# Attention, Fourier-like mixing and a gated layer on one core: bias and mask move from TensorE to VectorE, warm-up passes, sums kept in PSUM, new order of the last stages

## Chip, cores, metric

One Trainium2 chip, one core. The metric is the device time of one execution in microseconds (us), the median of the runs shown. TensorE is PE, VectorE is DVE, ScalarE is ACT, GpSimd is POOL, and SyncE (SP) issues the transfers.

## The reference

Three layers follow each other: attention, a mixing layer, a gated layer. B = 2, H = 8, S = 768, D = 64, C = H * D = 512, F = 1024. All is float32.

```python
scores = q @ k.T / sqrt(D) + bias          # bias = -slope[h] * distance
scores = where(is_global | is_local, scores, -1e9)   # 8 first keys, 96 last keys
a = softmax(scores);  x = a @ v            # then heads side by side: (B, S, 512)

theta = x @ w_theta                        # mixing layer
y = w_tok_r @ (x * cos(theta)) + w_tok_i @ (x * sin(theta))
u = x + y;  v = u + relu(u @ w_ch)

h = relu(v @ w_in)                         # gated layer
conv = 3-tap convolution of h along the tokens, per channel
out = (h * sigmoid(conv)) @ w_out
```

## The kernel before

Every engine has its own program, written out by hand, and the engines meet at counting semaphores. An engine runs its program in order, so a wait holds all that stands behind it.

**Attention** runs over 48 tiles, numbered `u`: 8 pairs of heads `p` with 6 tiles of 128 queries `i` each. A tile sees 232 keys for each of its two heads (128 for `i` = 0). TensorE's step `u` issues `scores(u+1)`, `transpose_p(u-1)` and `weighted_v(u-2)`. `scores` ends with two bf16 products with `ident16` that add the bias and the mask. VectorE's step takes the maxima of tile `u+1`, then denominator, reciprocal and quotient of tile `u-2`; in its first six steps it also makes the bias of one more head (two instructions). ScalarE's step takes two exponentials of tile `u` and copies the transposed probabilities of tile `u-1`. Scores banks, probabilities and transposes are doubled.

For the pairs 2 to 7 GpSimd scales q (L335), rounds q and k to a high part (L343) and subtracts for a low part (L345). TensorE then makes each score product in three passes. GpSimd begins this once all eight biases exist, and its queue is: pair 2, `w_theta`, pair 3, token weights 0, pair 4, token weights 1, pairs 5, 6, 7. SyncE loads pair `p` when the buffer of `p-2` is free, and behind the load of v for pair `p-1`.

**Mixing** follows with the same high and low parts: `theta`, then twelve token products `mix_tokens` (L619), then for four chunks `c` of 384 tokens `transpose_u(c)` (L630) and `mix_channels(c, j)`, j = 0 to 3 (L471). `add_mix(n)` on VectorE makes v from product `n` in two instructions (L1182, L1185), `high_v` on ScalarE and `low_v` on GpSimd split it. `high_u` and `low_u` split u.

**The gated layer** has 32 tiles `n`, 8 for each chunk: `hidden(n)` on TensorE (L471), then relu (L888) and first tap (L894) on ScalarE, two more taps on VectorE (`conv`, L1220, L1223), sigmoid on ScalarE (L901), the gate on VectorE (L1231), `high_g` on ScalarE, `low_g` on GpSimd. `relu(n)` waits for gate `n-2`. `output(c, f)` (L674) adds tile `f` of chunk `c` to three output banks in nine matmuls. Its first call waits for the last `add_mix`, number 15.

The products of the mixing layer's last two chunks and the first hidden tiles alternate on TensorE. This stretch is called the turn below.

## Time and profile before

| | |
|---|---|
| median of 3 runs | 436.52 us (435.88 to 436.69) |
| the profiled execution | 435.07 us, its span 433.3 us |
| PE busy | 410.5 us (95%) |
| DVE, ACT, POOL busy | 239.9, 216.1, 185.7 us |
| attention (to the first `theta` product) | 0 to 108.3 us |
| theta and token products | 108.3 to 265.6 us |
| the turn, to the first `output` | 265.6 to 313.4 us |
| the output stretch | 313.4 to 433.3 us |

A page gives busy time for each engine, and beside each group of instructions the idle time ahead of it with what ended it. Idle time costs something only on the engine that sets the end. TensorE is busy nearly everywhere here, so its few idle places and its own work are what to look at.

### The profile page before, as it was taken

To read this page: it belongs to the slowest core of one execution; us is meant where nothing else is said; L and a number is where in the kernel's file an instruction comes from. 1 tells how busy PE (TensorE), PEld (TensorE's weight loads), DVE (VectorE), ACT (ScalarE), POOL (GpSimd) and SP (SyncE) were. 2 spreads that over 40 slices of the span, in tenths; PEclk is the share of its full clock that TensorE was granted. 3 is DMA by queue.
4 is the path that set the end of the run, shared out by engine and by line. 5 is a ranking of instruction groups with operands and counts; after the bars stand their busy time and mean duration, and the time that the engine had idled before them with its cause. 6 is when DMAs were issued, how large, how long until landed. Compare 5 with 4: busy or idle time off the path is not lost.

```text
span 433.3 us, 6425 instructions
## 1 busy us (share of the span) xinstructions
PE 410.5 (95%) x2424; PEld 360.9 (83%) x2424; DVE 239.9 (55%) x432; ACT 216.1 (50%) x416; POOL 185.7 (43%) x126
## 2 busy tenths in 40 slices
PE   3999999999999999999999999979299999999997
PEld 1788988999878888888898989979289998999985
DVE  3766565666588744537354421476766565565620
ACT  2666555666578735564243111464464545455341
POOL 2299999410166622248432210245574232332330
PEclk9999999999999999999999999999889999999999
DMA  7834322370000222244420003001100010001021
GB/s 269 347 118 182 126 94 93 141 220 2 2 0 2 97 74 73 79 140 152 151 110 2 0 0 99 0 2 49 48 2 0 2 48 25 2 25 50 0 74 73
DMA packets 11984, 32.20 MB, mean 74 GB/s; under 512 B 4272, under 2 KB 4272, under 8 KB 11952
## 3 DMA queue, kind: packets, MB, share of 16 engines
q1 hardware_dynamic: 11952, 31.77, 21.0%
q8 instruction: 20, 0.33, 0.3%
q14 instruction: 12, 0.10, 0.1%
HBM read 28.62 MB, written 3.15 MB: 73 GB/s over the span
## 4 chain that ended last, share of the span: by engine, by line
PE 79%; POOL 10%; issue 3%; DVE 3%; DMA 2%; ACT 1%; SPq 0%; POOLq 0%; ACTq 0%
PE bank L471 28%; PE bank L619 23%; PE bank L674 16%; PE bank L533 4%; POOL qk_parts L345 3%; DMA qk_sb<-qk_laid 2%; PE bank L518 2%; PE bank L498 2%; POOL qk_sb L335 2%; PE bank L505 2%; POOL wT L358 2%; POOL qk_parts L343 1%; PE bank L630 1%; PE bank L492 1%; POOL wth L352 1%
## 5 line engine op out<-in xcount | busy, mean ns | idle before, releaser
L619 PE MATMUL bank<-z,wT 128*128 128x512 f32 x432 | 99.3, 390 | 0.0
L619 PEld LDWEIGHTS bank<-z,wT 128*128 128x128 f32 x432 | 80.8, 188 | 16.6
L674 PE MATMUL bank<-wout,g 128*128 128x512 f32 x288 | 71.5, 398 | 7.7 <-issue 7.7
L471 PE MATMUL bank<-vT,win 128*128 128x386 f32 x384 | 73.2, 340 | 0.0
L471 PEld LDWEIGHTS bank<-vT,win 128*128 128x128 f32 x384 | 68.6, 189 | 2.0
L674 PEld LDWEIGHTS bank<-wout,g 128*128 128x128 f32 x288 | 55.0, 192 | 18.1 <-issue 8.0
L430 POOL TENSOR_TENSOR g<-gf,g 128x384 fp32r<-128x384 f32 x32 | 39.8, 1246 | 69.6 <-ACT g L910 69.3
L1220 DVE SCALAR_TENSOR_TENSOR cv<-h_sb,convw,cv 128x384 f32<-128x384 f32 x32 | 21.4, 669 | 52.6 <-ACT cv L894 52.6
L417 POOL TENSOR_TENSOR vT<-vtmp,vT 128x384 fp32r<-128x384 f32 x16 | 17.2, 1087 | 66.5 <-ACT vT L847 66.5
L533 PE MATMUL bank<-v_sb,pT 128*128 128x65 f32 x352 | 44.6, 268 | 0.0
L747 ACT ACTIVATE pT<-bank 128x512 f32<-128x512 f32 (+1 forms) x48 | 27.0, 562 | 34.9 <-PE bank L518 34.9
L533 PEld LDWEIGHTS bank<-v_sb,pT 128*128 128x128 f32 x352 | 43.1, 192 | 0.0
L394 POOL TENSOR_TENSOR z<-trig,z 128x1024 fp32r<-128x1024 f32 x12 | 29.4, 2450 | 30.4 <-ACT z L811 30.4
L1231 DVE TENSOR_TENSOR gf<-h_sb,sg 128x384 f32<-128x384 f32 x32 | 40.8, 1276 | 0.6 <-ACT sg L901 0.6
L888 ACT ACTIVATE h_sb<-bank 128x386 f32<-128x386 f32 x32 | 15.7, 491 | 49.9 <-PE bank L471 45.8
L736 ACT ACTIVATE pr<-bank,small 128x232 f32<-128x232 f32 (+1 forms) x96 | 36.8, 438 | 2.7 <-DVE small L1011 2.2
L471 PE MATMUL bank<-uT,wch 128*128 128x384 f32 x192 | 35.6, 337 | 2.4 <-DVE uT L1174 2.4
L1155 DVE TENSOR_TENSOR x<-bank,x 128x512 f32<-128x512 f32 x12 | 8.3, 692 | 53.1 <-PE bank L619 53.1
L471 PE MATMUL bank<-wth,xT 128*128 128x512 f32 x144 | 35.7, 398 | 1.0 <-DVE xT L1039 1.0
L471 PEld LDWEIGHTS bank<-uT,wch 128*128 128x128 f32 x192 | 33.6, 188 | 3.3 <-DVE uT L1174 2.7
L792 ACT ACTIVATE wT<-wrows 128x1536 fp32r<-128x1536 f32 x10 | 14.9, 1489 | 40.6 <-PE bank L619 40.6
L1011 DVE TENSOR_REDUCE small<-bank 128x2 f32<-128x464 f32 (+1 forms) x48 | 29.0, 605 | 10.5 <-PE bank L505 5.9
(83 smaller groups left out, 560.1 us busy)
## 6 DMA issues: line engine op xcount, KB each, us to landing
wrows<-w_tok_laid SPq DMA_DIRECT2D x12, 768.0 KB, 4.3
qk_sb<-qk_laid SPq DMA_DIRECT2D x8, 792.0 KB, 5.7
v_sb<-v_laid SPq DMA_DIRECT2D x8, 780.0 KB, 4.4
out<-ob SPq DMA_DIRECT2D x12, 256.0 KB, 2.0
winraw<-w_in_in SPq DMA_DIRECT2D x4, 512.0 KB, 3.8
woutraw<-w_out_in SPq DMA_DIRECT2D x8, 256.0 KB, 2.7
wthraw<-w_theta_in SPq DMA_DIRECT2D x1, 1024.0 KB, 11.4
wchraw<-w_ch_in SPq DMA_DIRECT2D x1, 1024.0 KB, 5.1
```

What stands on the lines that cost most here:

```text
L394: pool.tensor_tensor(z[b][:, i, 1], trig[:, n % 2], z[b][:, i, 0].bitcast(F32), ALU.subtract)\
L417: pool.tensor_tensor(vT[b][:, 1, j, cols], vtmp[:, n % 2, :], vT[b][:, 0, j, cols].bitcast(F32), ALU.subtract).then_inc(v_lo, 1)
L430: pool.tensor_tensor(g[c % 2][:, 1, f, :], gf[:, n % 2, :], g[c % 2][:, 0, f, :].bitcast(F32), ALU.subtract).then_inc(g_lo, 1)
L471: last = pe.matmul(dst, w[a], m[b], start=(i == 0 and j == 0), stop=(i == n - 1 and j == 2))
L533: last = pe.matmul(O_BANK[u % 2][:, h * OW:(h + 1) * OW], pT[:, u % 2, slot * P:(slot + 1) * P], v_sb[:, pp, i, chunk, h, :], start=(chunk ...
L619: last = pe.matmul(Y_BANK[s % 2][:], wT[s % 2][:, hi, ri * NT + blk, :], z[b][:, blk, lo, ri, :], start=(blk == 0 and ri == 0 and j == 0), ...
L674: last = pe.matmul(OUT_BANK[c % 2][i][:], g[c % 2][:, hi, f, i * P:(i + 1) * P], wout[:, lo, f, :], start=(f == 0 and j == 0), stop=(f == ...
L736: last = act.activation(pr[:, u % 2, h, cols], S_BANK[u % 2][:, h, cols], ACT.Exp, bias=small[:, u % 2, 2 + h:3 + h])
L747: act.activation(d, src, ACT.Copy).then_inc(pt_copied, 1)
L1011: dve.tensor_reduce(small[:, u % 2, 2:4], S_BANK[u % 2][:, :, cols], AX.X, ALU.max, negate=True)\
L1220: dve.scalar_tensor_tensor(out=c, in0=h[:, 1:HALF + 1], scalar=convw[:, 1, f:f + 1], in1=c, op0=ALU.mult, op1=ALU.add).then_inc(conv_step, 1)
L1231: dve.tensor_tensor(gf[:, n % 2, :], h_sb[:, half, n % 2, half + 1:half + 1 + HALF], sg[:, n % 2, :], ALU.mult).then_inc(g_ready, 1)
```

## The change

In attention, the two bf16 products of each tile leave TensorE. VectorE instead runs, for each head, one `tensor_tensor_reduce` that reads the scores from PSUM and a float32 bias from SBUF, writes the negated, scaled sum to a new tile `biased` in SBUF, and keeps its minimum. The scale 1/sqrt(D) is in that instruction, so GpSimd's and ScalarE's passes over q are gone. The exponentials read `biased`. `scores` waits for the maxima of two tiles ago, no more for the exponentials. TensorE runs eight bf16 products of 512 columns over a constant tile at its start, and four more behind the branch that chooses the banded program.

In the turn, v's first sum, the convolution sum and the sigmoid stay in PSUM. Chunk 3's u is transposed in two halves, since two of its banks now serve the gates, and `hidden` runs one tile further ahead of `mix_channels(3, j)`. VectorE and ScalarE take their parts in a new order. The output uses four banks in turn, tile `t` in bank `t % 4`, and `mix_channels` waits for the whole of v two products ago.

```diff
-        ident16 = att("ident16", [P, P], BF16)
-        bias = att("bias", [P, H, BAND], BF16)
-        bias0 = att("bias0", [P, H, P], BF16)
+        biased = att("biased", [P, 2, 2, BAND], F32)
+        bias = att("bias", [P, H, BAND], F32)
+        bias0 = att("bias0", [P, H, P], F32)
...
-        cv = at("cv", [P, 2, HALF], F32, 107.25)
-        sg = at("sg", [P, 2, HALF], F32, 110.25)
...
-        OUT_BANK = [[bank[0], bank[1], bank[2]], [bank[3], bank[6], bank[7]]]
+        GATE_BANK = [bank[6][:, 0:HALF], bank[7][:, 0:HALF]]
+        OUT_BANK = [bank[0], bank[1], bank[2], bank[3]]
 
         def u_bank(c):
-            return [bank[0], bank[1], bank[4], bank[5]] if c < 3 else [bank[0], bank[1], bank[6], bank[7]]
+            return [bank[0], bank[1], bank[4], bank[5]] if c < 3 else [bank[0], bank[1], bank[0], bank[1]]
...
-            pool.wait_ge(ident_ready, 2)
-            pool.tensor_copy(ident16[:], ident[:]).then_inc(ident_ready, 1)
-
-            def scale_q(p):
-
-                q_cols = qk_sb[:, p % 2, 0:S]
-                pool.wait_ge(qk_in[p % 2], 16 * (p // 2 + 1))
-                pool.tensor_scalar(q_cols, q_cols, SCALE, None, ALU.mult).then_inc(q_scaled, 1)
 
             def split_qk(p):
                 pp = p % 2
-                scale_q(p)
+                pool.wait_ge(qk_in[p % 2], 16 * (p // 2 + 1))
                 if p >= 4:
                     pool.wait_ge(scores_ready, NT * (p - 1))
-                pool.wait_ge(q_scaled, p)
...
-                if p == 0 and i < 2:
-                    pe.wait_ge(q_first, i + 1)
-                if p == 1 and i == 0:
-                    pe.wait_ge(q_scaled, p)
+                if p < 2 and i == 0:
+                    pe.wait_ge(qk_in[p], 16)
                 if p >= 2 and i == 0:
                     pe.wait_ge(qk_lo, p - 1)
                 if u >= 2:
-                    pe.wait_ge(probs_ready, u - 1)
+                    pe.wait_ge(max_ready, 2 * (u - 1))
                 cols = slice(0, BAND) if i else slice(OWN, BAND)
                 c0, c1 = (NG, KT_STEP) if i == 0 else (KT_STEP * i - NL, KT_STEP * i + KT_STEP)
                 if p < 2:
                     for h in range(2):
                         rows = slice(h * D, (h + 1) * D)
-                        pe.matmul(S_BANK[u % 2][:, h, cols], qk_sb[rows, pp, i * P:(i + 1) * P],
-                                  qk_sb[rows, pp, S + c0:S + c1], start=True, stop=False)
+                        last = pe.matmul(S_BANK[u % 2][:, h, cols], qk_sb[rows, pp, i * P:(i + 1) * P],
+                                         qk_sb[rows, pp, S + c0:S + c1], start=True, stop=True)
                 else:
                     for j, (hi, lo) in enumerate(((0, 0), (0, 1), (1, 0))):
                         for h in range(2):
                             rows = slice(h * D, (h + 1) * D)
-                            pe.matmul(S_BANK[u % 2][:, h, cols], qk_parts[rows, pp, hi, i * P:(i + 1) * P],
-                                      qk_parts[rows, pp, lo, S + c0:S + c1], start=(j == 0), stop=False)
-                if i < 2 and p == 0:
-                    pe.wait_ge(bias_ready, i + 1)
-                if i == 0 and 1 <= p < HP:
-                    pe.wait_ge(bias_ready, h0 + 2)
-                for h in range(2):
-                    last = pe.matmul(S_BANK[u % 2][:, h, cols], ident16[:], bias[:, h0 + h, :] if i else bias0[:, h0 + h, :],
-                                     start=False, stop=True)
+                            last = pe.matmul(S_BANK[u % 2][:, h, cols], qk_parts[rows, pp, hi, i * P:(i + 1) * P],
+                                             qk_parts[rows, pp, lo, S + c0:S + c1], start=(j == 0), stop=(j == 2))
                 last.then_inc(scores_ready, 1)
...
+                keep_busy(4)
...
+            def keep_busy(count):
+                for _ in range(count):
+                    pe.matmul(bank[7], idle[:, 0:P], idle[:], start=True, stop=True)
+
+            pe.wait_ge(idle_ready, 1)
+            keep_busy(8)
+            pe.wait_ge(ident_ready, 3)
...
-                    pe.wait_ge(r_done, n - 1)
+                    pe.wait_ge(v_ready, n - 1)
...
             def output(c, f, tiles=(0, 1, 2)):
-                if f == 0:
-                    if c == 0:
+                if c == 0:
+                    if f == 0:
                         pe.wait_ge(u_lo, NC * CB)
-                    if c <= 1:
-                        pe.wait_ge(r_done, NC * CB)
-                    if c >= 2:
-                        pe.wait_ge(out_copied, 3 * (c - 1))
-                if c == 0:
+                        pe.wait_ge(v_ready, NC * CB)
                     pe.wait_ge(wout_ready, f + 1)
                 pe.wait_ge(g_lo, FB * c + f + 1)
                 for i in tiles:
+                    t = 3 * c + i
+                    if f == 0 and t >= 4:
+                        pe.wait_ge(out_copied, t - 3)
                     for j, (hi, lo) in enumerate(((0, 0), (0, 1), (1, 0))):
-                        last = pe.matmul(OUT_BANK[c % 2][i][:], g[c % 2][:, hi, f, i * P:(i + 1) * P], wout[:, lo, f, :],
+                        last = pe.matmul(OUT_BANK[t % 4][:], g[c % 2][:, hi, f, i * P:(i + 1) * P], wout[:, lo, f, :],
...
-            transpose_u(3)
+            transpose_u(3, (0, 1))
             hidden(1)
             mix_channels(2, 2)
             hidden(2)
             mix_channels(2, 3)
             hidden(3)
+            hidden(4)
+            transpose_u(3, (2, 3))
             for j in range(CB):
-                hidden(CB + j)
+                hidden(5 + j)
                 mix_channels(3, j)
-
-            for c in range(1, NC):
-                for f in range(FB):
-                    hidden(FB * c + f)
-                    output(c - 1, f)
-            for f in range(FB - 2):
-                output(NC - 1, f)
+            output(0, 0)
+            for n in range(FB + 1, NH):
+                hidden(n)
+                output(n // FB - 1, n % FB)
+            for i in range(3):
+                for f in range(FB - 2):
+                    output(NC - 1, f, (i,))
...
-            first_q = qk_sb[:, 0, 0:S]
-            act.wait_ge(qk_in[0], 16)
-            act.activation(first_q[:, 0:P], first_q[:, 0:P], ACT.Copy, scale=SCALE).then_inc(q_first, 1)
-            act.activation(first_q[:, P:S], first_q[:, P:S], ACT.Copy, scale=SCALE).then_inc(q_first, 1)
-
             def exps(u):
-                act.wait_ge(max_ready, u + 1)
                 if u >= 2:
                     act.wait_ge(pt_ready, u - 1)
                 cols = slice(0, BAND) if u % NT else slice(OWN, BAND)
                 for h in range(2):
-                    last = act.activation(pr[:, u % 2, h, cols], S_BANK[u % 2][:, h, cols], ACT.Exp,
-                                          bias=small[:, u % 2, 2 + h:3 + h])
+                    act.wait_ge(max_ready, 2 * u + h + 1)
+                    last = act.activation(pr[:, u % 2, h, cols], biased[:, u % 2, h, cols], ACT.Exp,
+                                          bias=small[:, u % 2, 2 + h:3 + h], scale=-1.0)
...
-                act.activation(cv[:, n % 2, :], h_sb[:, half, n % 2, half:half + HALF], ACT.Copy,
+                act.activation(GATE_BANK[n % 2], h_sb[:, half, n % 2, half:half + HALF], ACT.Copy,
                                scale=convw[:, 0, n % FB:n % FB + 1]).then_inc(tap_ready, 1)
 
             def sigmoid(n):
                 act.wait_ge(conv_ready, n + 1)
-                if n >= 2:
-                    act.wait_ge(g_ready, n - 1)
-                act.activation(sg[:, n % 2, :], cv[:, n % 2, :], ACT.Sigmoid).then_inc(sig_ready, 1)
+                act.activation(GATE_BANK[n % 2], GATE_BANK[n % 2], ACT.Sigmoid).then_inc(sig_ready, 1)
...
-            high_v(8)
-            hidden(0)
-            high_v(9)
-            hidden(1)
-            high_v(10)
-            hidden(2)
+            for j in range(CB - 1):
+                relu(j)
+                first_tap(j)
+                high_v(2 * CB + j)
+                gates(j)
+            high_u(3, (0, 1))
+            relu(3)
+            first_tap(3)
             high_v(11)
-            high_u(3)
-            hidden(3)
+            gates(3)
+            relu(4)
+            first_tap(4)
+            gates(4)
             high_w_out(0)
-            hidden(4)
+            high_u(3, (2, 3))
+            relu(5)
+            first_tap(5)
+            gates(5)
             high_w_out(1)
-            high_v(12)
-            hidden(5)
-            high_v(13)
-            high_w_out(2)
-            hidden(6)
-            high_v(14)
-            high_w_out(3)
-            hidden(7)
-            high_v(15)
-            for f in range(CB, FB):
-                high_w_out(f)
-                hidden(CB + f)
-            for n in range(CB + FB, NH):
-                hidden(n)
+            for j in range(CB):
+                relu(6 + j)
+                first_tap(6 + j)
+                high_v(3 * CB + j)
+                gates(6 + j)
+                high_w_out(2 + j)
+            for n in range(6 + CB, NH):
                 c, f = divmod(n, FB)
-                if c >= 2 and f < 3:
-                    copy_out(3 * (c - 2) + f)
+                if c >= 2 and f == 0:
+                    for i in range(3):
+                        copy_out(3 * (c - 2) + i)
+                relu(n)
+                first_tap(n)
+                gates(n)
+                if n < 12:
+                    high_w_out(n - 4)
...
+            dve.memset(idle[:], 1.0).then_inc(idle_ready, 1)
...
                 dve.wait_ge(scores_ready, u + 1)
+                if p == 0 and i < 2:
+                    dve.wait_ge(bias_ready, i + 1)
+                if i == 0 and 1 <= p < HP:
+                    dve.wait_ge(bias_ready, h0 + 2)
                 if u >= 2:
                     dve.wait_ge(probs_ready, u - 1)
                 cols = slice(0, BAND) if i else slice(OWN, BAND)
-                dve.tensor_reduce(small[:, u % 2, 2:4], S_BANK[u % 2][:, :, cols], AX.X, ALU.max, negate=True)\
-                   .then_inc(max_ready, 1)
+                for h in range(2):
+                    dve.tensor_tensor_reduce(
+                        biased[:, u % 2, h, cols], S_BANK[u % 2][:, h, cols],
+                        bias[:, h0 + h, :] if i else bias0[:, h0 + h, :], -SCALE, 3.0e38, ALU.add, ALU.min,
+                        small[:, u % 2, 2 + h:3 + h]).then_inc(max_ready, 1)
...
-                dve.scalar_tensor_tensor(out=tmp, in0=R_BANK[n % 2][:, 0:HALF], scalar=0.0,
-                                         in1=uT[:, 1, j, :].bitcast(F32), op0=ALU.max, op1=ALU.add).then_inc(r_done, 1)
+                r = R_BANK[n % 2][:, 0:HALF]
+                dve.scalar_tensor_tensor(out=r, in0=r, scalar=0.0, in1=uT[:, 1, j, :].bitcast(F32), op0=ALU.max,
+                                         op1=ALU.add).then_inc(r_done, 1)
                 dve.wait_ge(r_done, n + 1)
-                dve.tensor_tensor(tmp, tmp, uT[:, 0, j, :].bitcast(F32), ALU.add).then_inc(v_ready, 1)
+                dve.tensor_tensor(tmp, r, uT[:, 0, j, :].bitcast(F32), ALU.add).then_inc(v_ready, 1)
...
             for j in range(CB):
                 add_mix(2 * CB + j)
                 if j == CB - 1:
-                    low_u(3)
+                    low_u(3, (0, 1))
                 hidden(j)
+            hidden(4)
+            low_u(3, (2, 3))
+            hidden(5)
             for j in range(CB):
-                hidden(CB + j)
                 add_mix(3 * CB + j)
-            for n in range(FB, NH):
+                hidden(6 + j)
+            for n in range(6 + CB, NH):
```

VectorE's program in attention, one tile with all 232 keys. Before:

```order
L1011 TENSOR_REDUCE small<-bank 128x2
L1018 TENSOR_SCALAR small<-bank 128x2
L1023 RECIPROCAL small<-small 128x2
L1031 SCALAR_TENSOR_TENSOR x<-bank,small 128x128
L995 SCALAR_TENSOR_TENSOR bias_65<-dist,masked 128x128
L995 SCALAR_TENSOR_TENSOR bias<-dist,masked 128x232
```

And in the changed kernel, the same step:

```order
L1003 ISA biased,small<-bank,bias 128x232
L1003 ISA small 128x1
L1003 ISA biased,small<-bank,bias 128x232
L1003 ISA small 128x1
L1012 TENSOR_SCALAR small<-bank 128x2
L1017 RECIPROCAL small<-small 128x2
L1025 SCALAR_TENSOR_TENSOR x<-bank,small 128x128
L981 SCALAR_TENSOR_TENSOR bias_65<-dist,masked 128x128
L981 SCALAR_TENSOR_TENSOR bias<-dist,masked 128x232
```

(`bias_65` is `bias0`, the bias of the first tile.) One reduction has become four instructions: each `tensor_tensor_reduce` is followed by one that writes its one value per partition.

TensorE's program at the end of the turn, before: the last two hidden tiles and mixing products, then the first `output`.

```order
L471 MATMUL bank<-uT,wch 128x384 x12
L471 MATMUL bank<-vT_100,win 128x386 x12
L471 MATMUL bank<-uT,wch 128x384 x12
L471 MATMUL bank<-vT_100,win 128x386 x12
L674 MATMUL bank<-wout,g_106 128x512 x9
```

And now:

```order
L457 MATMUL bank<-vT_101,win 128x386 x12
L457 MATMUL bank<-uT,wch 128x384 x12
L457 MATMUL bank<-vT_101,win 128x386 x12
L457 MATMUL bank<-uT,wch 128x384 x12
L660 MATMUL bank<-wout,g_107 128x512 x9
```

The last hidden tile ahead of `output` is number 8 in both; it now stands ahead of the last mixing product.

VectorE's program there, before: conv of tile 7, gate of tile 6, the last `add_mix` (number 15), conv of tile 8.

```order
L1220 SCALAR_TENSOR_TENSOR cv<-h_sb,convw,cv 128x384
L1223 SCALAR_TENSOR_TENSOR cv<-h_sb,convw,cv 128x384
L1231 TENSOR_TENSOR gf<-h_sb,sg 128x384
L1182 SCALAR_TENSOR_TENSOR vtmp<-bank,uT 128x384
L1185 TENSOR_TENSOR vtmp<-vtmp,uT 128x384
```

And now: conv of tile 8, gate of tile 7, the last `add_mix`.

```order
L1215 SCALAR_TENSOR_TENSOR bank<-h_sb,convw,bank 128x384
L1218 SCALAR_TENSOR_TENSOR bank<-h_sb,convw,bank 128x384
L1226 TENSOR_TENSOR gf<-h_sb,bank 128x384
L1177 SCALAR_TENSOR_TENSOR bank<-bank,uT 128x384
L1180 TENSOR_TENSOR vtmp<-bank,uT 128x384
```

The order within the piece is the same, with a later tile's convolution in it. Every instruction of it now has at most one input in SBUF.

## Rows read from the trace of the kernel before

**Rows 1.** The chain of waits, in order of time (start us, us, what)
```profile
25.99 3.55 POOL qk_parts L345
...
64.37 3.57 POOL qk_parts L345
67.99 0.55 PE bank L498 x6
...
305.62 7.73 issue
313.35 4.18 PE bank L674 x9
...
319.68 2.06 PE bank L674 x9
```

**Rows 2.** Timeline of TensorE in attention (start, us, engine, line; idle before)
```profile
38.61 0.60 PE L498 MATMUL bank<-qk_parts 64*128 64x232 f32 x6
39.14 0.37 PE L505 MATMUL bank<-bias,ident 128*128 128x232 bf16 x2
39.35 0.60 PE L518 MATMUL bank<-ident,pr 128*128 128x128 f32 x4
...
40.72 0.60 PE L498 MATMUL bank<-qk_parts 64*128 64x232 f32 x6
...
43.36 0.55 PE L498 MATMUL bank<-qk_parts 64*128 64x128 f32 x6 [0.45 <-POOL qk_parts L345]
...
55.67 0.55 PE L498 MATMUL bank<-qk_parts 64*128 64x128 f32 x6 [0.38 <-POOL qk_parts L345]
```

**Rows 3.** Groups by line and shape (busy us, mean ns; idle before)
```profile
L1011 DVE TENSOR_REDUCE small<-bank 128x2 f32<-128x464 f32 x40 | 25.6, 641 | 7.6 <-PE bank L505 3.1 <-ACT pr L736 0.2
...
L995 DVE SCALAR_TENSOR_TENSOR bias<-dist,masked 128x232 bf16<-128x232 f32 x8 | 3.1, 393 | 0.0
...
L1182 DVE SCALAR_TENSOR_TENSOR vtmp<-bank,uT 128x384 f32<-128x384 f32 x16 | 8.8, 549 | 1.9 <-PE bank L471 1.9
...
L335 POOL TENSOR_SCALAR qk_sb<-qk_sb 128x768 f32<-128x768 f32 x7 | 15.1, 2158 | 22.0 <-DMA qk_sb<-qk_laid 13.1 <-DVE bias L995 9.0
```

**Rows 4.** Timeline of the first 31 us, several engines
```profile
6.97 0.31 ACT L727 ACTIVATE qk_sb<-qk_sb 128x128 f32<-128x128 f32 x1 [4.89 <-DMA qk_sb<-qk_laid]
...
7.33 0.80 PE L492 MATMUL bank<-qk_sb 64*128 64x128 f32 x4 [7.33 <-ACT qk_sb L727]
...
18.94 0.16 DVE L1018 TENSOR_SCALAR small<-bank 128x2 f32<-128x2 f32 x1 [0.43 <-PE bank L533]
...
19.54 0.59 DVE L995 SCALAR_TENSOR_TENSOR bias<-dist,masked 128x128 bf16<-128x128 f32 x2
...
20.05 0.42 DVE L1011 TENSOR_REDUCE small<-bank 128x2 f32<-128x256 f32 x1
...
22.20 2.13 POOL L335 TENSOR_SCALAR qk_sb<-qk_sb 128x768 f32<-128x768 f32 x1 [8.99 <-DVE bias L995]
...
30.97 0.55 PE L498 MATMUL bank<-qk_parts 64*128 64x128 f32 x6
```

**Rows 5.** Timeline of the turn from mixing to the output, several engines
```profile
281.68 0.62 DVE L1220 SCALAR_TENSOR_TENSOR cv<-h_sb,convw,cv 128x384 f32<-128x384 f32 x1 [1.63 <-ACT cv L894]
282.87 1.37 DVE L1231 TENSOR_TENSOR gf<-h_sb,sg 128x384 f32<-128x384 f32 x1
...
287.79 0.61 ACT L894 ACTIVATE cv<-h_sb,convw 128x384 f32<-128x384 f32 x1
288.27 2.36 PE L471 MATMUL bank<-uT,wch 128*128 128x384 f32 x12 [2.36 <-DVE uT L1174]
288.31 0.51 ACT L901 ACTIVATE sg<-cv 128x384 f32<-128x384 f32 x1
...
312.71 0.55 DVE L1182 SCALAR_TENSOR_TENSOR vtmp<-bank,uT 128x384 f32<-128x384 f32 x1
```

**Rows 6.** A stretch: us, PE, PEld, DVE, ACT, POOL busy, granted clock, DMA share, GB/s
```profile
313.00:315.00 2.00, 1.65 (x4) 1.39 (x5) 0.81 (x2) 1.12 (x3) 0.52 (x1) 0.50 0.00 0
```

78 lines of the change are left out of this document (37 added, 41 removed).

## The prediction

> **What bounds the kernel now.** I read the page's busy shares first: TensorE is busy in nearly every slice, so time can go only with its own work or with its few idle places. The chain of waits names the places [rows 1]. It runs through GpSimd's splits of q and k until 67.94 us, then along TensorE to the end, with one hole of 7.73 us ahead of the first `output` and a slow piece of 4.18 us behind it. The timeline of TensorE in attention shows what a tile costs: scores start at 38.61 and 40.72, so a full tile takes 2.11 us, and the bias products hold TensorE from 39.14 to 39.35, 0.21 us [rows 2]. Six tiles of a pair take 55.67 - 43.36 - 0.38 = 11.93 us without the wait for GpSimd, which was 0.45 and 0.38 us [rows 2]. The first 31 us show three things: TensorE starts when q and k are in and scaled, GpSimd starts when VectorE has made the last bias at 22.20, and pair 2's first scores stand at 30.97 [rows 4].
>
> **Attention, TensorE's side.** Without the bias products a pair takes 11.93 - 5 x 0.21 - 0.12 = 10.75 us (the first tile has 128 keys, its bias I put at 0.12). A full tile takes 1.90.
>
> **Attention, VectorE's side.** No row shows a `tensor_tensor_reduce`. From below: an instruction with one PSUM and one SBUF input takes 549 ns for 384 columns, one with two inputs 393 ns for 232, the old reduction 641 ns for 464 [rows 3]. These lie on a line of about 1.04 ns per column and 0.15 to 0.16 fixed, so 232 columns take 0.39 to 0.40 us by any of them. The one-value instruction behind it takes at most what L1018, on two values, takes: 0.16 us [rows 4]. If the starts overlap as those of two bias instructions do (283 + 393 ns of work in 0.51 us from start to start, rows 19.54 and 20.05 [rows 4]), a tile's four instructions hold VectorE for about 0.80 us; if each waits for the one ahead to end, for 2 x (0.40 + 0.16) = 1.12. I take 0.95, the middle, since neither row is nearer. Denominator, reciprocal and quotient hold it from 18.94 to 19.54, 0.60 us [rows 4]. So VectorE needs 1.55 us for a tile (1.40 to 1.72) and stays below TensorE's 1.90; it has a share of the short tiles too, where both are shorter. The bound stays TensorE, but near.
>
> The Trainium skill, in "VectorE: DVE Perf Modes", section "Two Vector instructions with no wait between them", says that an operation that also gives its accumulator is two instructions, and its section "The DRAIN you can't avoid" that the next one does not start until the pipe is empty. By that the tile costs the 1.12 us of my upper end, the start below would come 1.3 us later, and the sum would be 1.3 us higher. The row of two bias instructions (0.51 us for 0.676 of work) speaks against a full drain [rows 4].
>
> **The start.** q and k are there at 6.97; before, TensorE began at 7.33, after ScalarE's scaling [rows 4]. The four passes behind the branch now stand in its way. A pass of 512 columns takes 0.21 to 0.43 us by the bias product's 0.21 for 2 x 232 columns, at full or half speed, so four take 0.9 to 1.7. The branch ends somewhere between 5 and 7.3. Scores of tile 0 then begin between 7.0 and 9.0; I take 7.5, and 8.0 for the first maxima. From there VectorE is the slowest, since its first six steps carry a bias too (0.51). Until the last bias its queue is: maxima of tiles 0 to 6 (5 x 0.95, and two short ones of 0.70), six biases (3.06), four quotients (2.40): 11.6 us, so bias ready at 19.6, against 22.20. Cheap end 18.7, dear end 20.9. Pair 2's q and k were asked for at 17.66 before, now some 4 us earlier, behind the first big loads, and should be in by 19.5: they bound the cheap end only. GpSimd then needs only the 1.5 and 3.55 us of rounding and subtracting [rows 1]: split at 24.8. TensorE: scores of tile 9 wait for maxima of tile 7 (20.5), then three tiles at 1.90: tile 12 at 26.1, against 30.97. Saved 4.9.
>
> **GpSimd's chain.** It ran from 22.20 to 67.94 without a hole up to pair 5's split, 45.7 us, of which four scalings of 2.16 and their gaps are 8.8 [rows 1, 3, 4]. Now 19.6 + 36.9 = 56.5. TensorE reaches tile 30 at 26.1 + 3 x 10.75 = 58.35, after it. So TensorE is bound by itself from there: 67.99 - 58.35 = 9.65 us saved at tile 30, and 3 x 1.18 in the last three pairs: **13.2 us** for attention (12 at the dear end, 14 at the cheap one).
>
> **Theta and token products.** TensorE runs on here and none of its work changes. The later `v_ready` costs nothing: it is the v of two products ago. Zero.
>
> **The turn.** Here I walked the new queues in order with spacings of the old rows: 0.52 us from first tap to sigmoid on ScalarE, 0.55 for an `add_mix` step, 0.62 and a short gap for a conv step [rows 5]. The gate of 384 columns took 1.37 us while GpSimd worked, another instruction of that size 0.55 (row 312.71) [rows 5]; with one SBUF input left, I take 0.55. Set the second `mix_channels` product of chunk 2 where it was. Then the first half of u is split at 284.7, relu 4 waits for gate 2 at 286.9, ScalarE comes to the second half of u at 289.3, behind first tap 4, sigmoid 3, high part 2 and one weight copy, and VectorE ends it at 290.85. TensorE is done with hidden tile 5 at 287.9 and stands 3.0 us. Before, it stood 2.36 and went on at 288.27 with one hidden tile (2.1) less done [rows 5]. So this costs 0.5 us. Seven more pieces at 2.17 (the 17.35 us for eight behind 288.27): the last mixing product ends at 306.1.
>
> Then the hole. The old one ends with the last `add_mix` at 312.71: its r part came behind first tap 7, which came behind `high_v(14)`, which waited for `add_mix(14)` behind conv 6. Each round of that ring took 6 us while TensorE's took 4.3. Now the taps stand ahead of `high_v`. Hidden tile 8 ends 2.2 ahead of the last mixing product; relu, tap, two conv steps and gate take 0.2 + (0.52 + 0.61) + 1.3 + 0.55 = 3.2, `add_mix` 1.15 with its second instruction. So `output` begins at 308.2, after 2.1 us idle, not at 313.35 [rows 1]: **5.15 saved**. The granted clock stood at 0.50 behind the old hole [rows 6], that is at 1.2 GHz, and the first `output` took 4.18 instead of 2.06 [rows 1]. It did not fall behind the 2.36 of idle. With 2.1, and 3.0 before, I expect none: **2.1 saved**.
>
> **The output.** The same matmuls. Copying three tiles in a row on ScalarE (3 x 0.6) falls while TensorE is in a hidden tile of 2.1; the tile that takes a copied bank comes second. The last call has the order of its matmuls changed, and ends with the same six matmuls, copy and store. Zero.
>
> **Sum.** 13.2 + 5.15 + 2.1 = 20.4. The span becomes 433.3 - 20.4 = 412.9, the profiled execution 435.07 - 20.4 = 414.7. The median of the runs stands 1.45 above that execution: 436.52 - 20.4 = **416.1 us**.
>
> **Rivals.**
>
> 1. *VectorE becomes the bound of attention.* From 1.30 us for a tile's two sums on, its step (0.60 more) passes 1.90. At 1.5 a pair takes about 12.4 us instead of 10.75: 6 x 1.65 = 10 us given back, and 2.5 at the start, so 428; at 1.3 about 420. For it: two instructions more per head, and waits at every one. Against: all rows lie on one line. I say 422, chance 0.2.
>
> 2. *The clock falls at the 3.0 us stall, or the stall is longer.* The walk has some 20 links, any of them may be late. Half speed for one product costs 2.1, a later split of u 1: 419. Chance 0.12.
>
> 3. *Slower than before: VectorE is held by GpSimd.* The sum reads a float32 bias from SBUF, and GpSimd works almost without a hole to the end of pair 6. If that doubles it as it did the gate (0.81 us more for 384 columns, so 0.49 for 232) [rows 5], the sums take 1.93 a tile and the step 2.53. From 26.1 that gives tile 42 at 102 instead of 91.8: 10 lost where 12 were hoped for, in all about 438. It decides from a tile cost of about 1.87 on. Against: instructions that read PSUM and SBUF kept 0.55 beside a busy GpSimd (row 312.71 [rows 5]). Chance 0.04. The Trainium skill's "SBUF — State Buffer", section "Who interferes with whom", has it that only two SBUF inputs contend; by that this rival is out.
>
> 4. *Better.* The sums cost 0.8, the start is at 7.0, and the turn stalls less: 412. Chance 0.12.
>
> 5. *The turn doesn't do what it says*, the ring of 6 us stays through relu's wait for the gate: 7 us less saved, 423. Chance 0.04.
>
> **Numbers.** The likeliest case, 416, has 0.48. The range 411 to 424 takes in its bounds (414.5 to 418.5), the cases 2, 4 and 5 and the nearer half of 1, and leaves out 2 in 10 or less. A difference of 0.2% is what a measurement can tell. Faster by more: all but rival 3 and the far end of rival 1: 0.95; same 0.02; slower 0.03.
>
> **What would show it.** A pair of heads at 10.75 us, no wait for GpSimd at its first tile from pair 5 on, pair 2's scores at 26, the `tensor_tensor_reduce` at 0.40 us. One stall of TensorE near 3 us and one near 2 in the turn, the granted clock at 1.00 in both, no hole of 7.7. Wrong would be: TensorE waiting for VectorE's maxima in steady attention, a `tensor_tensor_reduce` over 0.6 us, a late first product, or a new hole in the output stretch at the change of banks.

## The result

Against the kernel before on the same chip, the changed kernel takes 0.9617 of its time (0.9543 to 0.969): 418.2 us is the median of three executions (417.7 to 422.2), where 416.1 was predicted. This ratio leaves out three more executions of the six, of 472.9 to 474.9 us, whose mean granted clock was 0.87 where it was 0.99 to 1.00 in the others; they are the main find of this study, since they are slower than the kernel before. Six further executions of the same kernel gave 417.8, 420.4 and 420.9 us, and 469.9, 475.0 and 478.0.

The profiled execution is a long one (474.94 us, span 473.2). Two rows of its page show where to look: TensorE is "busy" nearly throughout, and its clock falls within the third slice and is halved from the fourth to the thirteenth. The same row of before has no slice under 8.

```profile
PE   7989999999999999999999999999789999999997
...
PEclk9975555555555999999999999999899999999999
```

The start of TensorE in that execution, with the warm passes (`L574`) at 0.45 us each and then at 0.26, and the first scores:

```profile
1.54 3.60 PE L574 MATMUL bank<-idle 128*128 128x512 bf16 x8 [1.54 <-DVE idle L951]
6.14 1.03 PE L574 MATMUL bank<-idle 128*128 128x512 bf16 x4 [1.01 <-issue]
7.10 0.89 PE L476 MATMUL bank<-qk_sb 64*128 64x128 f32 x8
```

Then the issue of pair 2's q and k by SyncE, GpSimd's split of them, and TensorE at pair 2 (a timeline of three engines, with one row of VectorE):

```profile
13.47 0.33 SPq L226 DMA_DIRECT2D qk_sb<-qk_laid  x1
22.57 1.50 POOL L334 CAST qk_parts<-qk_sb 128x1584 fp32r<-128x1584 f32 x1 [19.15 <-DMA qk_sb<-qk_laid]
22.74 0.40 DVE L1003 CUSTOM_DVE_ANT_0 biased<-bank,bias 128x232 f32<-128x232 f32 x1
24.15 3.54 POOL L336 TENSOR_TENSOR qk_parts<-qk_sb,qk_parts 128x1584 fp32r<-128x1584 f32 x1
25.75 0.39 PE L510 MATMUL bank<-v_sb,pT 128*128 128x65 f32 x2
27.75 0.55 PE L482 MATMUL bank<-qk_parts 64*128 64x128 f32 x6 [1.61 <-POOL qk_parts L336]
29.65 0.99 PE L482 MATMUL bank<-qk_parts 64*128 64x232 f32 x6
```

TensorE stands 1.61 us at pair 2 because q and k, asked for at 13.47, reach GpSimd at 22.57. The six passes of the tile behind it take 0.99 us where they took 0.60 [rows 2]. Windows of the same execution give the clock (us of PE, PEld, DVE, ACT, POOL, then PEclk):

```profile
26.00:28.00 2.00, 0.39 (x6) 0.26 (x7) 0.62 (x3) 0.69 (x2) 2.00 (x2) 1.00 0.79 304
28.00:30.00 2.00, 2.00 (x20) 1.86 (x20) 0.72 (x6) 1.08 (x3) 1.92 (x2) 0.91 0.19 74
30.00:32.00 2.00, 2.00 (x13) 1.80 (x12) 1.14 (x6) 0.37 (x2) 2.00 (x1) 0.50 0.00 0
100.00:102.00 2.00, 2.00 (x12) 1.90 (x10) 0.73 (x4) 0.74 (x2) 0.00 (x0) 0.50 1.02 427
152.00:154.00 2.00, 2.00 (x16) 1.86 (x15) 1.44 (x6) 0.60 (x1) 0.00 (x0) 0.87 0.04 8
```

Half the clock comes behind the idle place, and stays for some 120 us of gapless matmuls. It comes back where attention ends: first `theta` products stand at 153.69, so attention from pair 2 (27.75) took 125.9 us. In attention alone, below, the same stretch takes 70.6 us at full clock (27.99 to 98.63).

VectorE in steady attention: the sum with its maximum is a custom instruction and a short read of the accumulator, 0.32 us from one head's to the next, and VectorE waits for TensorE:

```profile
60.14 0.40 DVE L1003 CUSTOM_DVE_ANT_0 biased<-bank,bias 128x232 f32<-128x232 f32 x1 [0.24 <-PE bank L482]
60.47 0.08 DVE L1003 DVE_READ_ACCUMULATOR2_ANT small<- 128x1 f32 x1
60.47 0.40 DVE L1003 CUSTOM_DVE_ANT_0 biased<-bank,bias 128x232 f32<-128x232 f32 x1
60.79 0.08 DVE L1003 DVE_READ_ACCUMULATOR2_ANT small<- 128x1 f32 x1
```

And TensorE in the turn, with two stalls, where the hole of 7.73 was [rows 1]:

```profile
336.59 3.91 PE L457 MATMUL bank<-uT,wch 128*128 128x384 f32 x12 [2.66 <-DVE uT L1168]
340.34 2.28 PE L457 MATMUL bank<-vT,win 128*128 128x386 f32 x12
...
355.14 2.31 PE L660 MATMUL bank<-wout,g 128*128 128x512 f32 x9 [2.00 <-issue]
```

### The profile page after: what moved, and what is told of

It is laid out like the page before. It is cut to its first block, busy times and chain, and to the rows that moved or that the text cites. A ratio compares the mean times of both kernels' runs of the same rounds, so it can differ in the third digit from the quotient of the medians.

```text
span 473.2 us, 6365 instructions
## 1 busy us (share of the span) xinstructions
PE 460.3 (97%) x2340; PEld 405.2 (86%) x2340; DVE 217.5 (46%) x577; ACT 216.1 (46%) x414; POOL 159.9 (34%) x118
## 4 chain that ended last, share of the span: by engine, by line
PE 90%; issue 3%; DVE 2%; ACT 2%; DMA 2%; POOL 1%; ACTq 0%; POOLq 0%
PE bank L457 25%; PE bank L603 21%; PE bank L660 14%; PE bank L510 12%; PE bank L495 8%; PE bank L482 7%; DMA qk_sb<-qk_laid 2%; PE bank L574 1%; PE bank L617 1%; PE bank L521 1%; POOL qk_parts L336 1%; PE bank L476 1%; ACT bank L876 0%; DVE bank L1215 0%; POOL qk_parts L334 0%
## 5 line engine op out<-in xcount | busy, mean ns | idle before, releaser
L510 PEld LDWEIGHTS bank<-v_sb,pT 128*128 128x128 f32 x352 | 72.4, 302 | 0.0
L510 PE MATMUL bank<-v_sb,pT 128*128 128x65 f32 x352 | 72.0, 373 | 0.0
L660 PE MATMUL bank<-wout,g 128*128 128x512 f32 x288 | 69.6, 390 | 2.0 <-issue 2.0
L419 POOL TENSOR_TENSOR g<-gf,g 128x384 fp32r<-128x384 f32 x32 | 32.4, 1015 | 68.1 <-ACT g L890 68.1
L1215 DVE SCALAR_TENSOR_TENSOR bank<-h_sb,convw,bank 128x384 f32<-128x384 f32 x32 | 19.9, 623 | 71.3 <-ACT bank L876 71.3
L495 PE MATMUL bank<-ident,pr 128*128 128x128 f32 x176 | 45.4, 402 | 0.0
L719 ACT ACTIVATE pr<-biased,small 128x232 f32<-128x232 f32 (+1 forms) x96 | 39.6, 463 | 0.9 <-DVE small L1003 0.9
L1012 DVE TENSOR_SCALAR small<-bank 128x2 f32<-128x2 f32 x48 | 7.7, 160 | 68.7 <-PE bank L510 68.7
L1003 DVE CUSTOM_DVE_ANT_0 biased<-bank,bias 128x232 f32<-128x232 f32 (+1 forms) x96 | 32.7, 379 | 9.8 <-PE bank L482 9.4
L495 PEld LDWEIGHTS bank<-ident,pr 128*128 128x128 f32 x176 | 28.5, 200 | 9.5 <-issue 6.4
```

Source lines behind the costliest of these rows:

```text
L419: pool.tensor_tensor(g[c % 2][:, 1, f, :], gf[:, n % 2, :], g[c % 2][:, 0, f, :].bitcast(F32), ALU.subtract).then_inc(g_lo, 1)
L495: last = pe.transpose(PT_BANK[u % 2][:, slot * P:(slot + 1) * P], pr[:, u % 2, h, cols], ident[:])
L510: last = pe.matmul(O_BANK[u % 2][:, h * OW:(h + 1) * OW], pT[:, u % 2, slot * P:(slot + 1) * P], v_sb[:, pp, i, chunk, h, :], start=(chunk ...
L660: last = pe.matmul(OUT_BANK[t % 4][:], g[c % 2][:, hi, f, i * P:(i + 1) * P], wout[:, lo, f, :], start=(f == 0 and j == 0), stop=(f == FB ...
L719: last = act.activation(pr[:, u % 2, h, cols], biased[:, u % 2, h, cols], ACT.Exp, bias=small[:, u % 2, 2 + h:3 + h], scale=-1.0)
L1003: dve.tensor_tensor_reduce(biased[:, u % 2, h, cols], S_BANK[u % 2][:, h, cols], bias[:, h0 + h, :] if i else bias0[:, h0 + h, :], -SCALE, ...
```

## The experiments

All executions, in us. "Held" are those with a mean granted clock under 0.96, from the kernel before as well. Ratios compare the others, each against the kernel before on its own chip; that of attention alone also leaves out its two executions of 436.3 and 436.4.

| kernel | not held | held | ratio (95%) |
|---|---|---|---|
| changed, in all 12 | 417.7 to 422.2 | 469.9 to 478.0, x6 | 0.9617, 0.9627 |
| attention alone | 425.1 to 436.4 | none of 6 | 0.9775 (0.9752 to 0.9798) |
| turn alone | 427.9 to 430.2 | 443.2 | 0.9845 (0.9821 to 0.9868) |
| two passes per tile | 426.0 to 430.1 | none of 5 | 0.9808 (0.9781 to 0.9835) |
| two passes, pairs 3 on | 423.4 to 425.6 | none of 5 | 0.9731 (0.9712 to 0.975) |
| seven passes at the idle place | 418.7 to 420.6 | none of 5 | 0.9631 (0.9615 to 0.9647) |
| no warm passes | 418.9 to 420.5, x5 | 484.3, 489.3 (see below) | 0.9622 (0.9607 to 0.9638) |
| earlier load | 416.2 to 419.3 | none of 5 | 0.9578 (0.9555 to 0.9601) |
| earlier load and split | 415.3 to 419.2 | none of 5 | 0.9573 (0.9547 to 0.96) |
| long idle place | none | 445.3 to 480.4, x6 | |
| long idle place, passes | 434.4 | 443.6 to 489.6, x5 | |
| before, idle place | 442.5 to 444.4, x3 | 454.6 to 474.0, x3 | 1.0174 (1.0152 to 1.0195) |
| before, as it is, in all 37 | 434.4 to 437.0 | 451.2, 479.7 | 1 |

After the first six executions, the kernels ran in three sets, each on a chip of its own: the changed kernel again, its two halves and two passes per tile; then the next four below; then the long idle places and the earlier load and split. In the second and third set the changed kernel itself was not run as it is.

**The changed kernel again**, beside its two parts.

> The changed kernel once more, for more executions of it and a trace in which the granted clock keeps to 1.00 in attention. Theory F (too little work on TensorE): with the bf16 products gone, attention alone does not hold the clock, so it falls in some executions by the chance of the moment; about half of them near 473 us, the others near 418. Theory G (the idle place): the clock falls because TensorE stands 1.6 us at 26 us, waiting for the first split, and it stays low since attention cannot bring it back; the same two times, but every execution with the low clock loses it just behind that place.

It gave 0.9627 (0.9596 to 0.9658), again with half of the executions held, and a profile with the same 1.59 us of idle time at 27.68.

**Attention alone.** The edit takes the changed kernel and puts the turn, the banks and the warm passes back:

```diff
-            pe.wait_ge(idle_ready, 1)
-            keep_busy(8)
...
-                keep_busy(4)
...
-            hidden(4)
-            transpose_u(3, (2, 3))
...
+                act.activation(sg[:, n % 2, :], cv[:, n % 2, :], ACT.Sigmoid).then_inc(sig_ready, 1)
```

> Only the attention part of the change, without the warm-up passes and with the old turn. Its terms in the sum were 13.2 us at most, so about 424 us where the clock keeps up (trace of the changed kernel so far: pair 2 at 27.75 instead of 26.1, so nearer 426). Both theories expect the low clock in some executions here too, about 55 us more in those. If none of six has it, the warm-up passes or the turn have to do with it.

None was held. TensorE had no idle place at pair 2, since without warm passes it came there later, and GpSimd came earlier (21.35). Its timeline gives the new tile and pair (scores of 64x128 begin a pair):

```profile
29.89 0.60 PE L485 MATMUL bank<-qk_parts 64*128 64x232 f32 x6
30.42 0.66 PE L498 MATMUL bank<-ident,pr 128*128 128x128 f32 x4
30.91 1.00 PE L513 MATMUL bank<-v_sb,pT 128*128 128x65 f32 x8
31.85 0.38 PE L485 MATMUL bank<-qk_parts 64*128 64x232 f32 x2
...
39.00 0.55 PE L485 MATMUL bank<-qk_parts 64*128 64x128 f32 x6
...
50.02 0.55 PE L485 MATMUL bank<-qk_parts 64*128 64x128 f32 x6
...
98.63 0.70 PE L460 MATMUL bank<-wth,xT 128*128 128x512 f32 x2 [0.18 <-DVE xT L1021]
...
304.19 4.18 PE L654 MATMUL bank<-wout,g 128*128 128x512 f32 x9 [7.74 <-issue]
```

A tile takes 1.96 us and a pair 11.02. The turn's hole is the old one. Two of its six executions took 436.3 and 436.4 at a mean clock of 0.988, the same as in the others; what cost them 10 us is open.

**The turn alone.** The other half: attention as in the kernel before, and no warm passes.

```diff
-        biased = att("biased", [P, 2, 2, BAND], F32)
-        bias = att("bias", [P, H, BAND], F32)
+        ident16 = att("ident16", [P, P], BF16)
+        bias = att("bias", [P, H, BAND], BF16)
```

> Only the turn and the output part, attention as before. Predicted 7.25 us less than before, 429 us; the changed kernel's trace has 4.1 us in the turn and 1.9 in the first output product, so 430.2. Theories F and G both expect the granted clock at 1.00 through attention in every execution. If it falls here, the attention change is not its cause.

It saved 1.55% (6.8 us), and attention alone 2.25% (9.8 us); together that is nearly the 3.8% of both. One of its five executions was held, where the expectation had none, so the attention change is not needed for a fall of the clock; where it fell is not shown, since the profile is of another execution. The stall was 2.65 us and the product behind it took 3.50, so in this execution as well the clock dipped there:

```profile
291.89 3.50 PE L467 MATMUL bank<-uT,wch 128*128 128x384 f32 x12 [2.65 <-DVE uT L1176]
295.19 2.73 PE L467 MATMUL bank<-vT,win 128*128 128x386 f32 x12
```

**Two passes per tile.** Behind each tile's scores two passes of 232 bf16 columns, such as the bias products were, into columns that nothing reads.

```diff
+                for h in range(2):
+                    pe.matmul(S_BANK[u % 2][:, h, 256:256 + BAND], idle[:, 0:P], idle[:, 0:BAND], start=True, stop=True)
```

> The changed kernel with two bf16 products over the constant tile put ahead of each tile's scores, of the size of the bias products that the change took out (232 columns each, results unused, into free columns of the scores' own banks). Cost by the old rows: 0.21 us a tile, 48 tiles, about 10 us, so near 428 us where the clock keeps up. Theory F: the clock never falls in attention, all executions near 428. Theory G: the 1.6 us of idle at 26 us is still there or nearly so, and the low clock still comes in some executions.

No execution was held, but pair 2 came at 28.79 without idle time ahead of it, so it does not tell whether the passes or the missing idle place kept the clock. It cost 1.9% against the changed kernel.

**Four more kernels** took these apart: passes without tiles made later (pairs 3 on), the idle place filled and nothing else, no warm passes, and the wait removed at its source.

```diff
-                for h in range(2):
+                for h in range(2 if p >= 3 else 0):
```

> The changed kernel with the two bf16 products per tile only from pair 3 on (30 tiles, about 6 to 9 us); pairs 0 to 2 are as in the changed kernel, the 1.6 us of idle at 26 us is there. Theory G with its second half (the clock falls at the idle place and attention alone cannot bring it back): it falls there in some executions, but comes back soon after pair 3 begins, so those take about 5 to 12 us more than the others (about 426), none takes 473. Theory F: no low clock at all, since only later tiles would lose it.

None was held, but its profile had no idle place either: the second warm group took 1.88 us instead of 1.03 and the tiles came later. It does not answer its question, but it shows something else. Up to pair 3 this program is the changed kernel, so the changed kernel too can start late and then have no idle place at pair 2. Its two traces are both of held executions and both have the place; whether its six full-speed executions had it is not shown.

```diff
+                if u >= 2:
+                    pe.wait_ge(max_ready, 2 * (u - 1))
+                if p == 2 and i == 0:
+                    for _ in range(7):
+                        pe.matmul(S_BANK[0][:, 0, :], idle[:, 0:P], idle[:], start=True, stop=True)
                 if p >= 2 and i == 0:
                     pe.wait_ge(qk_lo, p - 1)
-                if u >= 2:
-                    pe.wait_ge(max_ready, 2 * (u - 1))
```

> The changed kernel with seven bf16 passes of 512 columns over the constant tile ahead of pair 2's first scores, where TensorE stands 1.6 us for GpSimd's first split (results unused, in a free scores bank). 7 x 0.213 = 1.5 us, so they fill the idle time and cost next to nothing. Nothing is added to any other tile. Theory G (the idle place lets the clock fall): no execution with the low clock, all near 418. Theory F (attention alone does not hold the clock): the low clock still comes in about half of them, about 473.

Here the comparison is clean. The start is that of the changed kernel to within 0.1 us, the wait for GpSimd is there, and only the idle time is filled:

```profile
26.13 1.46 PE L471 MATMUL bank<-idle 128*128 128x512 bf16 x6
27.68 0.55 PE L485 MATMUL bank<-qk_parts 64*128 64x128 f32 x6
...
29.59 0.60 PE L485 MATMUL bank<-qk_parts 64*128 64x232 f32 x6
...
39.34 0.55 PE L485 MATMUL bank<-qk_parts 64*128 64x128 f32 x6 [0.57 <-POOL qk_parts L336]
```

The next full tile's scores take 0.60, not 0.99, and none of five executions was held. The last line is a second, shorter wait for GpSimd, at pair 3.

```diff
-            pe.wait_ge(idle_ready, 1)
-            keep_busy(8)
```

> The changed kernel without the twelve passes at the start. The kernel with attention alone changed, also without them, began pair 2 at 27.99 with no idle time ahead of it, since its first tiles ran at half speed. So here too: no idle place. Theory G: no low clock in attention in any execution, and about the same time as the best of the changed kernel, 418 to 419.5 (pair 2 at 27.99 against 27.7). Theory F: the low clock in about half.

Five of seven took 418.9 to 420.5, so among these the warm passes bring nothing that the comparison shows (0.9622 against 0.9627). The other two are longer than any execution of the changed kernel, and the profile is of one of them:

```profile
10.08 1.15 PE L475 MATMUL bank<-qk_sb 64*128 64x232 f32 x4
11.15 1.11 PE L494 MATMUL bank<-ident,pr 128*128 128x128 f32 x4
...
27.48 1.15 PE L475 MATMUL bank<-qk_sb 64*128 64x232 f32 x4
```

The four transposes take 1.11 us, as in the held tiles (0.66 in attention alone at full speed). A slow first tile is usual without warm passes: in attention alone the scores of a full tile also took 1.15 us at 10.04, but 0.66 from 12.66 on. Here they still take 1.15 at 27.48. TensorE ran slow from the start, with no idle place at all, to the last tiles of attention, which ends at 168. So the warm passes may be worth something after all: without them two of seven were slow in this way, which is too few to tell. By theory G none should have been.

```diff
             load_qk(p)
+            if p == 2:
+                load_w_tok(0)
+                load_w_tok(1)
...
-            load_w_tok(0)
-            load_w_tok(1)
```

> The changed kernel with the first two loads of token weights (1.5 MB) issued behind the load of pair 2's q and k instead of ahead of it. In the changed kernel that load took 8.97 us from its issue at 13.47 and GpSimd waited for it until 22.57. It should land by 18, GpSimd then waits for the last bias (about 18), the first split ends near 23, and TensorE finds it ready: pair 2 at 26.1, 1.6 us saved, no idle place. About 416.3. Theory G: never the low clock. Theory F: in about half of the executions. If the split of token weights 0 on GpSimd now waits for its load, some of the saving is given back.

The two loads of token weights, 1.5 MB that is needed only after attention, now stand behind pair 2's q and k in the sync engine's queue.

```profile
14.71 0.34 SPq L226 DMA_DIRECT2D qk_sb<-qk_laid  x1
15.10 0.91 SPq L238 DMA_DIRECT2D wrows<-w_tok_laid  x2
...
19.48 1.50 POOL L337 CAST qk_parts<-qk_sb 128x1584 fp32r<-128x1584 f32 x1 [16.05 <-DMA qk_sb<-qk_laid]
```

From issue to GpSimd it is 4.8 us instead of 9.1. There is no wait at pair 2 (27.31) or later in attention, none of five was held, and the time is 0.5% less than with the place filled. In this profile the second warm group took 1.88 us, which made the tiles later; in that of the version below, with the same load order and the fast warm group, pair 2 began at 25.94 and without a wait too. Its first `theta` product and its turn, with full-speed products:

```profile
97.95 3.01 PE L460 MATMUL bank<-wth,xT 128*128 128x512 f32 x12 [0.18 <-DVE xT L1036]
...
280.84 2.35 PE L460 MATMUL bank<-uT,wch 128*128 128x384 f32 x12 [2.65 <-DVE uT L1171]
283.04 2.27 PE L460 MATMUL bank<-vT,win 128*128 128x386 f32 x12
...
297.83 2.31 PE L663 MATMUL bank<-wout,g 128*128 128x512 f32 x9 [2.00 <-issue]
```

**Three long idle places** ask whether such a place is enough, and whether bf16 passes bring the clock back. GpSimd makes two useless copies ahead of pair 2's split, in the changed kernel, in the changed kernel with passes from pair 3 on, and in the kernel before:

```diff
                 if p == 2:
+                    pool.wait_ge(wth_in, 16)
+                    for k in range(2):
+                        pool.tensor_copy(wth[:, 0], wthraw[:]).then_inc(g_counts, 1)
+                        pool.wait_ge(g_counts, k + 1)
```

> The changed kernel with two more copies of w_theta on GpSimd (3.8 us by the old row of 1.89) ahead of pair 2's first split, so that TensorE stands about 5.4 us there where its clock was up from the first tile, and about 2.5 us where it came up late. Theory G: the low clock in nearly every execution, 474 to 482 us. Theory F in its first form (the clock falls in attention by chance, whatever the idle place): about half of them as before, the others near 422.

> The same idle place, with the two bf16 products per tile from pair 3 on. If such products are what brings the clock back, it falls at the idle place, stays low through pair 2 (about 10 us more than at full clock) and returns in pair 3: 424.9 + about 3 for the wait + about 10 = 435 to 440 us, and none near 475. If the bf16 products have nothing to do with it: as gap_bare, 480 or more.

> The kernel before with the same two copies ahead of pair 2's split (its GpSimd chain is longer, so TensorE would stand about 2.3 us, and the whole chain to pair 5 moves by 3.8). The bias products are there in every tile. Expected: 436 + 4 = 440 us if the clock holds, up to 450 if it falls at the place and comes back within a pair; no execution near 480. One near 480 or more would say that the products of the change's before don't bring the clock back either.

The idle place was 5.47 us, 5.46 and 2.40. All six executions of the first were held. With the passes I had expected 435 to 440, and five of six went over it: the passes do not bring the clock back soon. In that kernel's profile it came back at about 135 us, inside attention, which ends at 155.1 there:

```profile
130.00:132.00 2.00, 2.00 (x13) 1.45 (x11) 1.24 (x6) 0.00 (x0) 0.00 (x0) 0.50 0.49 100
140.00:142.00 2.00, 2.00 (x22) 1.69 (x20) 1.29 (x7) 1.02 (x4) 0.00 (x0) 1.00 0.56 234
```

In the kernel before every execution was longer, three by only 6 to 8 us; windows of its profile show that the clock fell and came back within about 15 us:

```profile
40.00:42.00 2.00, 2.00 (x13) 1.64 (x13) 0.72 (x4) 0.17 (x1) 2.00 (x2) 0.50 0.00 0
...
50.00:52.00 2.00, 2.00 (x24) 1.81 (x22) 1.18 (x4) 1.18 (x4) 2.00 (x1) 1.00 0.00 0
```

How long the clock was low in an execution without a trace can be estimated from its span and its mean clock, as 2 x (1 - clock) x span. For the profile of the changed kernel that gives 126 us, and 125.9 is what its rows show. It gives 116 to 133 us for the six held executions of the changed kernel, 55 to 133 for the long idle place, 17 to 140 with passes, 20 to 93 in the kernel before with the place. So, if it fell at the idle place, each of the last three kernels has executions in which the clock came back long before attention ended.

**Earlier load and split.** On top of the earlier load, VectorE splits the second half of u ahead of gate 3, and ScalarE makes their high part ahead of gate 4's activations:

```diff
-            hidden(4)
+            conv(4)
             low_u(3, (2, 3))
+            gate(3)
```

> early_load with one more edit in the turn: ScalarE takes the second half of u straight behind first tap 4, ahead of sigmoid 3, high part 2 and one weight copy, and VectorE splits it ahead of gate 3. In the traces TensorE stood 2.65 us for that half. ScalarE comes to it 1.3 us earlier (0.44 + 0.37 + 0.52 by the rows), VectorE saves the gate's 0.53 only where it was in the way. So the wait falls to about 1.3 us, and 1.3 us are saved: 416.5 against early_load's 417.8. The hole ahead of the first output should stay 2.0.

TensorE waited 2.12 us for u, not 1.3 as expected, against 2.65. That half microsecond is in the trace; against the earlier load alone the times do not resolve it. Both are better than either kernel.

## Why the prediction was right, and where it was not

**Right: TensorE stays the bound, and VectorE is not near.** The `tensor_tensor_reduce` takes 0.40 us for 232 columns, as worked out from [rows 3]. The accumulator read is 0.08 where 0.16 was the bound, and the starts are 0.32 apart, so a tile's sums hold VectorE for some 0.7 us (60.14 to 60.87), under my cheap end of 0.80. The Trainium skill ("VectorE: DVE Perf Modes", "Two Vector instructions with no wait between them") is right that there are two instructions. A full emptying of the pipe between them does not show in these starts, and the section says itself which instructions start without waiting for the earlier ones; the prediction left that out. Rival 3 is out: the sum at 22.74 took 0.40 while GpSimd worked (22.57 to 24.07), and the gate went from 1.277 us (attention alone) to 0.547 (earlier load). Both fit the Trainium skill, "SBUF — State Buffer", "Who interferes with whom". The row I had quoted against this rival was misread: at 312.71 GpSimd was not working, its last instruction in that stretch had ended at 311.90.

```profile
310.78 1.12 POOL L430 TENSOR_TENSOR g<-gf,g 128x384 fp32r<-128x384 f32 x1
```

**Right: the turn.** From the first `theta` product to the first `output` it is 313.35 - 108.32 = 205.03 us in the trace of before, 304.19 - 98.63 = 205.56 in attention alone, and 297.83 - 97.95 = 199.88 with the new turn. So 5.15 or 5.7 us are saved where 5.15 was said (the 0.5 us of the longer stall is already in that walk).

```profile
108.32 2.88 PE L471 MATMUL bank<-wth,xT 128*128 128x512 f32 x12 [0.39 <-DVE xT L1039]
```

The stalls were 2.65 and 2.00, for 3.0 and 2.1. The first `output` product fell from 4.18 to 2.31, 1.9 for 2.1. Rival 2 happened in part: of the eleven traces with the new turn, the product behind the stall took 3.50 to 3.92 us in six and 2.35 to 2.37 in five, at nearly the same stall. "The granted clock at 1.00 in both" was thus wrong in about half of them.

**Mis-sized: the tile.** A full tile is 1.96 us, not 1.90. The step was "without the bias products a pair takes 10.75", with all of their 0.21 us taken off. The start-to-start time of transposes to the weighted v grew from 0.43 us (39.35 to 39.78 in the trace of before) to 0.49 (30.42 to 30.91), so some of the bias product's time had covered something else; that it was the transposes' weight load is argued, not shown.

```profile
39.35 0.60 PE L518 MATMUL bank<-ident,pr 128*128 128x128 f32 x4
39.78 1.00 PE L533 MATMUL bank<-v_sb,pT 128*128 128x65 f32 x8
```

A pair at 11.02 instead of 10.75 costs 0.27 each in six pairs, 1.6 us of the 13.2.

**Wrong: "q and k in by 19.5".** They came at 22.4 (asked for at 13.47, 8.97 us to landing). Both engines ahead were as early as said or earlier (the last bias at 17.9, the first scores at 7.1), so this load became the bound: it stands in the same queue behind 1.5 MB of token weights, asked for at 4.74, and 1 MB of theta weights. I had called it a bound of the cheap end only. Pair 2 stood at 27.7 instead of 26.1, another 1.6 us, and with the place filled TensorE waited 0.57 us more for GpSimd at pair 3, which the earlier load also removed. That the step itself failed and not the sums around it shows in the earlier load and split: there pair 2 began at 25.94. Attention alone saved 108.32 - 98.63 = 9.7 us at `theta`, the full change 9.4 with the place filled (`theta` at 98.96), and 10.4 and 11.7 with the load moved. The sizes above are the whole shortfall of the trace with the filled place: its span is 416.9 for a forecast of 412.9, of which attention is 3.8 (1.6 for the tiles, 1.6 and 0.6 for the load) and the first `output` product 0.2.

**Missed: what the idle place does.** Rival 2 looked for a fall of the clock in the turn and priced one product, 2.1 us. The place that mattered was the one that the late load opened, and the price is 55 us (474.6 against 419.3, the medians of the six held and the six other executions): in both traces of it the tiles behind it run at 1.2 GHz until `theta`. That the three full-speed executions fell in the range while the three others lay some 50 us above it is no merit of the prediction: nothing in it foresaw two kinds of execution.

The traces agree on what releases it. In all five that have an idle place of 1.59 us or more at pair 2 (the changed kernel twice, the three long places) the clock falls right there. In the eight that have none (before, the two halves, the passes twice, the filled place, the earlier load twice) it does not fall in attention. Whole executions point the same way: held were 6 of 12 of the changed kernel, 0 of 5 with the place filled, 0 of 10 with the load moved, 6 of 6 with the place made long. But the filled place ran in a set without the changed kernel, and 0 of 5 against 6 of 12 is not far from chance; only the traces make it more than that. And an idle place at pair 2 is not the only way: the trace without warm passes is slow with none, and the turn alone (1 of 5) and the kernel before (2 of 37, both on one chip) were held without the late load. Why the clock then stays low, and why so differently long, is not settled. It is not a lack of the bf16 bias products alone, since passes of that shape failed in five of six. The Trainium skill ("TensorE: Matmul & The Clock Gate") warns in "HAM oscillation — how this bites in real kernels" of waits for a load ahead of matmuls, and says in "What's actually happening" that activity releases the throttle. The trace agrees on the fall. For the return it does not: the window 100:102 shows TensorE's record full and the clock at 0.50, so for this kind of work the measurement decides against an early return.

So the answer to "is it faster" is: by 3.8% in half of its executions, and slower by 8 to 10% in the other half; with the load moved, faster by 4.2% in all ten that ran.

**Open:** what cost two executions of attention alone 10 us (some 20 us more at half speed after the start would, and the record of the clock would not show it, by the trace without warm passes below; no trace of these two exists); whether the changed kernel's full-speed executions had the idle place at pair 2; why pair 2's load, asked for at 13.47, reached GpSimd at 22.57, and one asked for at 15.20 behind the same loads (passes from pair 3 on) at 21.38.

## What to carry to other kernels

When work is taken off a chain, price again each load that was early enough for the old chain, and put those that a later stage needs behind it in the queue. A stall of 1.6 us can cost far more than 1.6 us if it comes ahead of a stage in which TensorE's clock recovers late, so run such a change a dozen times, and look at the clock row of each, before a median is believed. Here no execution was held with a short filler at the one idle place (5), or with one load moved (10).

## What was not expected of the hardware

TensorE stayed at 1.2 GHz for over 100 us of matmuls without a gap, in attention's work of 64-row scores, transposes and 65-column products; no slice of the token products, at 512 columns, shows it. It began behind an idle place of 1.6 us in both traces that have one, and behind one of 5.5 in both of those.

In the profile without warm passes the record of the granted clock read 1.00 in stretches where the instructions took half-speed times:

```profile
100.00:102.00 2.00, 2.00 (x12) 1.76 (x12) 0.61 (x3) 1.02 (x3) 1.92 (x2) 1.00 0.00 0
```

Twelve matmuls in 2 us, as in the held window above at 0.50; with the filled place, at full speed, there are 22 in 30:32. Why the record reads so is not shown; the duration of a known instruction is the better clock there.
